# Written-out lists for the first four iterations of a fused convolution and two-layer-pair kernel, with block 2's taps summed on GpSimd

## What is computed

```python
w = softmax(weight_gen over its 7 taps)            # per token and head
x = sum over k of w[..., k] * x_pad[token - 6 + k] # causal, per head of 24 columns
h = x @ w_in                                       # 192 -> 2048
P = a0 + a1*h + a2*h**2 + a3*h**3
Q = 1 + |b0|*|h| + |b1|*h**2
x = (P / (Q + 1e-6)) @ w_out                       # 2048 -> 192
xn = x / sqrt(mean(x*x) + 1e-6) * rms_g
g, v = xn @ w_gate, xn @ w_val                     # 192 -> 1536 each
out = (silu(g) * v) @ w2_out                       # 1536 -> 192
```

## Time and profile before

| | before |
|---|---|
| median of 3 runs | 1414.27 us (1414.18 to 1414.41) |
| the profiled execution's own time | 1415.13 us |
| its span, first to last instruction | 1413.3 us |
| granted TensorE clock, mean | 0.996 |
| PE busy | 1390.0 us (98%) |
| DVE busy | 1166.2 us (83%) |
| ACT busy | 1068.9 us (76%) |
| POOL busy | 378.2 us (27%) |
| chain that ended last | PE 91%, DVE 6%, ACT 2% |

### The profile page before, as it was taken

How to read it: one execution, slowest core, us unless ns; L and a number is a source line. 1 busy time by engine, 2 the same in 40 slices (tenths; PEclk the granted TensorE clock), 3 DMA queues, 4 the chain that set the end, 5 groups by cost and what they waited for, 6 DMA issues and landing times.

```text
span 1413.3 us, 21338 instructions
## 1 busy us (share of the span) xinstructions
PE 1390.0 (98%) x7488; PEld 1247.9 (88%) x7488; DVE 1166.2 (83%) x1521; ACT 1068.9 (76%) x1388; POOL 378.2 (27%) x273
## 2 busy tenths in 40 slices
PE   7979999999999999999999999999999999999999
PEld 6858889899898998989898988989999899898988
DVE  8999988888797888888888888888879788888622
ACT  5887879878787877878787787987878787777521
POOL 3331332404233240332414133240423324000000
PEclk9999999999999999999999999999999999999999
DMA  8301000000000000000000100000000000000000
GB/s 231 90 0 32 2 32 13 32 12 0 31 11 31 11 7 35 0 31 11 31 11 0 42 0 31 11 31 11 0 31 11 31 11 1 12 1 1 12 12 12
DMA packets 12661, 32.35 MB, mean 23 GB/s; under 512 B 1620, under 2 KB 7506, under 8 KB 12624
## 3 DMA queue, kind: packets, MB, share of 16 engines
q1 hardware_dynamic: 11744, 31.42, 7.1%
q10 hardware_dynamic: 880, 0.43, 0.1%
HBM read 25.55 MB, written 6.29 MB: 23 GB/s over the span
## 4 chain that ended last, share of the span: by engine, by line
PE 91%; DVE 6%; ACT 2%; issue 0%; DMA 0%; ACTq 0%; DVEq 0%
PE dn L775 40%; PE bank L766 10%; PE bank L767 10%; PE bank L768 10%; PE bank L769 10%; PE bank L770 10%; PE bank L784 2%; DVE num L688 1%; DVE num L701 1%; DVE num L685 1%; DVE den L696 1%; DVE den L686 1%; DVE num L707 1%; ACT num L547 0%; ACT seed L558 0%
## 5 line engine op out<-in xcount | busy, mean ns | idle before, releaser
L775 PE MATMUL dn<-dn_w,num 128*128 128x192 f32 x2048 | 374.4, 327 | 5.5 <-DVE num L707 5.5
L775 PEld LDWEIGHTS dn<-dn_w,num 128*128 128x128 f32 x2048 | 340.1, 190 | 12.1 <-DVE num L707 6.7
L545 ACT ACTIVATE den<-bank,coef 128x512 f32<-128x512 f32 x256 | 175.8, 687 | 175.9 <-PE bank L770 166.9
L775 PE MATMUL dn<-dn_w,glu 128*128 128x192 f32 x1536 | 279.6, 326 | 0.0
L685 DVE TENSOR_TENSOR num<-num,bank 128x512 f32<-128x512 f32 x256 | 174.7, 682 | 106.9 <-ACT num L547 105.8
L775 PEld LDWEIGHTS dn<-dn_w,glu 128*128 128x128 f32 x1536 | 255.0, 190 | 4.0
L701 DVE SCALAR_TENSOR_TENSOR num<-num,coef,seed 128x1024 f32<-128x1024 f32 x128 | 166.9, 1305 | 56.2 <-ACT seed L568 55.7
L547 ACT ACTIVATE num<-bank,coef 128x512 f32<-128x512 f32 x256 | 200.0, 781 | 0.0
L686 DVE SCALAR_TENSOR_TENSOR den<-den,coef,bank 128x512 f32<-128x512 f32 x256 | 189.6, 741 | 0.0
L688 DVE SCALAR_TENSOR_TENSOR num<-num,coef,bank 128x512 f32<-128x512 f32 x256 | 189.6, 741 | 0.0
L732 DVE TENSOR_TENSOR glu<-glu,bank 128x512 f32<-128x512 f32 x192 | 130.8, 681 | 66.1 <-PE bank L770 64.8
(11 more groups left out here) (126 smaller groups left out, 2028.3 us busy)
## 6 DMA issues: line engine op xcount, KB each, us to landing
x_in<-in_x_dram SPq DMA_DIRECT2D x14, 960.0 KB
out_dram<-y_out SPq DMA_DIRECT2D x15, 384.0 KB, 2.3
w_blk<-in_weight_gen_dram SPq DMA_DIRECT2D x14, 112.0 KB, 2.0
dn_w<-in_moe_w_out_dram SPq DMA_DIRECT2D x1, 1536.0 KB, 10.9
dn_w<-in_moe_w_out_dram SPq DMA_DIRECT2D x1, 1152.0 KB, 18.2
num<-in_moe_w_in_dram SPq DMA_DIRECT2D x1, 768.0 KB, 7.9
num<-in_moe_w_in_dram SPq DMA_DIRECT2D x2, 384.0 KB, 9.0
x_in<-in_x_dram SPq DMA_DIRECT2D x1, 768.0 KB
```

What stands on the lines that cost most here:

```text
L545: act.activation(chunk(den, c % 8), h, ACT.Abs, scale=B_RAW[:, 1:2])
L775: done = pe.matmul(banks[:, j // 2, j % 2 * D:(j % 2 + 1) * D], acts[:, j * P:(j + 1) * P], w, start=first and j % 2 == 0, stop=last, skip ...
```

## The change

- Iterations 0 to 3 get lists of their own (`PE_OPENING` and so on). The loop's lists start at iteration 4, and lose what only the opening used. An entry `up1 4 0 < up1 0 0` is step `up1` 4 of block 0, which waits until the bank's content `up1` 0 of block 0 is read.
- Block 2's taps are no longer added by PE: POOL adds them, and two `xpose` steps follow.
- `w_first` is loaded by SP's queue ahead of x, no longer by ACT's. SP no longer waits for x or for the zeros before it issues the weights' loads. The zeros of the halo are written by DVE for block 0 and by POOL for block 1, in one partition at a time.
- ACT issues its small loads after the first exponential.
- The low part of piece 3 moves from DVE to POOL (`third_low`), with a semaphore of its own, for which `up1` 4 of block 0 waits. The first `mul` no longer waits for all low parts, but comes after `third_low` in POOL's order.
- `up1` 0 of each block starts with x's first low part and waits for the second in front of its fourth matmul.

`DVE_PROGRAM`, `UP1_BANK`, `GATE_BANK` and the loop's order of what is kept are the same.

```diff
-tap1 0 0, down1 10 2, down2 1 3, down1 11 2, down2 2 3, value 3 3, gate 5 3, up1 4 1, value 4 3, up1 5 1,
-tap1 1 0, down1 12 2, down2 3 3, down1 13 2, value 5 3, up1 6 1, tap1 2 0, tap2 0 0, gate 6 3, up1 7 1, tap1 3 0,
-tap2 1 0, down2 4 3, down1 14 2, down2 5 3, down1 15 2,
-value 6 3, gate 7 3, value 7 3, gate 8 3, up1 8 1, tap1 4 0, tap2 2 0, up1 9 1, tap1 5 0, tap1 6 0, tap2 3 0,
-gate 9 3, up1 10 1, tap2 4 0, down2 6 3, down1 0 1,
+ down1 10 2, down2 1 3, down1 11 2, down2 2 3, value 3 3, gate 5 3, up1 4 1, value 4 3, up1 5 1,
...
+PE_OPENING = opening("""
+up1 0 0, up1 1 0, up1 2 0, up1 3 0, up1 4 0 < up1 0 0, up1 5 0 < up1 1 0, tap 0 1, tap 1 1, tap 2 1,
+up1 6 0 < up1 4 0, up1 7 0 < up1 5 0, up1 8 0 < up1 2 0, up1 9 0 < up1 6 0, up1 10 0 < up1 7 0,
+up1 11 0 < up1 3 0, tap 3 1, tap 4 1, up1 12 0 < up1 9 0, up1 13 0 < up1 11 0, up1 14 0 < up1 10 0, tap 5 1,
+tap 6 1, up1 15 0 < up1 8 0, down1 0 0, down1 1 0, down1 2 0, down1 3 0, down1 4 0, down1 5 0,
+up1 0 1 < up1 12 0, down1 6 0, down1 7 0, up1 1 1 < up1 14 0, down1 8 0, up1 2 1 < up1 15 0, down1 9 0,
+down1 10 0, up1 3 1 < up1 13 0, down1 11 0, up1 4 1 < up1 0 1, up1 5 1 < up1 1 1, up1 6 1 < up1 4 1, down1 12 0,
+up1 7 1 < up1 5 1, down1 13 0, up1 8 1 < up1 2 1, down1 14 0, down1 15 0, up1 9 1 < up1 6 1, up1 10 1 < up1 7 1,
+down1 0 1, up1 11 1 < up1 3 1, down1 1 1, down1 2 1, xnx 0 0 < up1 10 1, xnx 1 0 < up1 8 1, down1 3 1,
+up1 12 1 < up1 9 1, up1 13 1 < up1 11 1, gate 0 0 < xnx 0 0, gate 1 0 < xnx 1 0, down1 4 1, up1 14 1 < gate 0 0,
+down1 5 1, up1 15 1 < gate 1 0, value 0 0 < up1 12 1, down1 6 1, gate 2 0 < up1 13 1, down1 7 1,
+gate 3 0 < up1 14 1, down2 0 0, gate 4 0 < gate 2 0, value 1 0 < up1 15 1, value 2 0 < value 0 0,
+value 3 0 < gate 3 0, down2 1 0, xpose 0 2 < value 2 0, xpose 1 2 < gate 4 0, gate 5 0 < value 1 0, down1 8 1,
+down2 2 0, up1 0 2 < xpose 0 2, up1 1 2 < value 3 0, up1 2 2 < gate 5 0, down1 9 1, up1 3 2 < xpose 1 2,
+down1 10 1, up1 4 2 < up1 0 2, up1 5 2 < up1 1 2, down1 11 1, down2 3 0, down1 12 1, value 4 0 < up1 3 2,
+down1 13 1, value 5 0 < up1 2 2, up1 6 2 < up1 4 2, up1 7 2 < up1 5 2, down2 4 0, down1 14 1,
+gate 6 0 < value 4 0, down2 5 0, down1 15 1, value 6 0 < value 5 0, gate 7 0 < up1 6 2, gate 8 0 < up1 7 2,
+value 7 0 < gate 6 0, value 8 0 < gate 7 0, up1 8 2 < value 6 0, down2 6 0, down1 0 2, down2 7 0, down1 1 2,
+up1 9 2 < value 8 0, gate 9 0 < value 7 0, gate 10 0 < up1 8 2, gate 11 0 < gate 8 0, value 9 0 < gate 9 0,
+value 10 0 < gate 10 0, up1 10 2 < gate 11 0, value 11 0 < up1 9 2, up1 11 2 < value 9 0, up1 12 2 < value 11 0,
+down2 8 0, down1 2 2, xnx 0 1 < up1 10 2, down1 3 2, xnx 1 1 < value 10 0, down2 9 0, down1 4 2,
+up1 13 2 < up1 11 2, up1 14 2 < xnx 0 1, up1 15 2 < xnx 1 1, xpose 0 3 < up1 12 2, down2 10 0, down1 5 2,
+down2 11 0, down1 6 2, xpose 1 3 < up1 13 2, down1 7 2, gate 0 1 < up1 14 2, gate 1 1 < up1 15 2,
+value 0 1 < xpose 0 3, gate 2 1 < xpose 1 3, gate 3 1 < gate 0 1,
+""")
+
+ACT_OPENING = opening("""
+linear 0 0, linear 1 0, linear 2 0, linear 3 0, table 0 0, abs 0 0, linear 4 0, linear 5 0, abs 1 0, root 0 0,
+square 0 0, square 1 0, linear 6 0, linear 7 0, piece 4 0, linear 8 0, linear 9 0, abs 2 0, abs 3 0, root 1 0,
+linear 10 0, linear 11 0, square 2 0, square 3 0, exp 0 2, abs 4 0, abs 5 0, linear 12 0, linear 13 0,
+linear 14 0, x_high 0 1, linear 15 0, root 2 0, x_high 1 1, square 4 0, square 5 0, abs 6 0, abs 7 0, root 3 0,
+square 6 0, linear 0 1, piece 5 0, linear 1 1, linear 2 1, linear 3 1, abs 0 1, linear 4 1, square 7 0,
+linear 5 1, abs 1 1, root 0 1, square 0 1, piece 6 0, square 1 1, linear 6 1, abs 2 1, ss 0 0, piece 7 0,
+linear 7 1, linear 8 1, linear 9 1, abs 3 1, root 1 1, linear 10 1, linear 11 1, square 2 1, abs 4 1,
+xn_high 0 0, xn_high 1 0, abs 5 1, square 3 1, root 2 1, silu 0 0, linear 12 1, silu 1 0, linear 13 1,
+linear 14 1, linear 15 1, square 4 1, silu 2 0, silu 3 0, square 5 1, silu 4 0, abs 6 1, abs 7 1, root 3 1,
+x_high 0 2, x_high 1 2, square 6 1, silu 5 0, linear 0 2, linear 1 2, linear 2 2, exp 0 3, square 7 1,
+linear 3 2, linear 4 2, linear 5 2, abs 0 2, abs 1 2, root 0 2, abs 2 2, linear 6 2, square 0 2, linear 7 2,
+silu 6 0, ss 0 1, abs 3 2, silu 7 0, square 1 2, root 1 2, silu 8 0, linear 8 2, square 2 2, square 3 2,
+linear 9 2, silu 9 0, silu 10 0, silu 11 0, abs 4 2, linear 10 2, linear 11 2, xn_high 0 1, xn_high 1 1,
+linear 12 2, abs 5 2, root 2 2, linear 13 2, linear 14 2, linear 15 2, x_high 0 3, y 0 0,
+""")
+
+DVE_OPENING = opening("""
+horner 0 0, horner 1 0, horner 2 0, horner 3 0, horner 4 0, horner 5 0, qy 0 0, py 0 0, py 1 0, newton 0 0,
+horner 6 0, horner 7 0, qy 1 0, horner 8 0, peak 0 2, newton 1 0, horner 9 0, horner 10 0, horner 11 0, py 2 0,
+qy 2 0, qy 3 0, newton 2 0, py 3 0, inverse 0 2, newton 3 0, horner 12 0, horner 13 0, horner 14 0, horner 15 0,
+x_low 0 1, qy 4 0, x_low 1 1, py 4 0, qy 5 0, newton 4 0, py 5 0, py 6 0, qy 6 0, newton 5 0, newton 6 0,
+horner 0 1, horner 1 1, horner 2 1, horner 3 1, horner 4 1, horner 5 1, qy 7 0, py 7 0, qy 0 1, newton 7 0,
+qy 1 1, py 0 1, py 1 1, horner 6 1, newton 0 1, newton 1 1, horner 7 1, xn 0 0, horner 8 1, horner 9 1,
+horner 10 1, horner 11 1, xn_low 0 0, xn_low 1 0, py 2 1, qy 2 1, newton 2 1, qy 3 1, py 3 1, horner 12 1,
+newton 3 1, horner 13 1, peak 0 3, horner 14 1, glu 0 0, horner 15 1, py 4 1, qy 4 1, py 5 1, glu 1 0, glu 2 0,
+newton 4 1, qy 5 1, glu 3 0, newton 5 1, x_low 0 2, x_low 1 2, py 6 1, qy 6 1, horner 0 2, newton 6 1,
+horner 1 2, horner 2 2, horner 3 2, horner 4 2, horner 5 2, py 7 1, qy 7 1, glu 4 0, newton 7 1, inverse 0 3,
+glu 5 0, horner 6 2, horner 7 2, py 0 2, glu 6 0, qy 0 2, newton 0 2, xn 0 1, glu 7 0, py 1 2, qy 1 2, glu 8 0,
+newton 1 2, horner 8 2, qy 2 2, py 2 2, horner 9 2, glu 9 0, glu 10 0, glu 11 0, horner 10 2, newton 2 2,
+qy 3 2, horner 11 2,
+""")
+
+POOL_OPENING = opening("""
+mul 0 1, mul 1 1, mul 2 1, mul 3 1, mul 4 1, mul 5 1, low 0 0 < newton 0 0, mul 6 1 < newton 0 0,
+less 0 2 < newton 1 0, low 1 0 < newton 1 0, norm 0 2 < newton 3 0, mul 0 2 < newton 3 0, mul 1 2, mul 2 2,
+add 1 2, low 2 0 < newton 6 0, mul 3 2 < newton 6 0, add 2 2, mul 4 2, add 3 2, low 3 0, low 4 0 < py 1 1,
+rms 0 0, low 5 0 < newton 1 1, low 6 0 < newton 1 1, mul 5 2, add 4 2, low 7 0, mul 6 2, add 5 2,
+less 0 3 < newton 3 1, add 6 2, norm 0 3 < newton 7 1, mul 0 3, mul 1 3, mul 2 3 < py 0 2, rms 0 1,
+add 1 3 < newton 0 2, mul 3 3 < qy 1 2, add 2 3 < newton 1 2, mul 4 3 < py 2 2, add 3 3 < py 2 2, mul 5 3,
+add 4 3, mul 6 3, add 5 3 < qy 3 2,
+""")
+
+OPENED = 4
...
-ONCE = ("piece", "low", "table")
-ALONE = {"tap1": 1, "tap2": 2}
-FLIPPED_IN_SUMS = (0, 1, 2)
-FROM_BLOCK = {"peak": 2, "less": 2, "exp": 2, "inverse": 2, "norm": 2,
-              "mul": 1, "add": 3, "xpose": 3, "x_high": 1, "x_low": 1}
 LAG = {(name, n): lag for name, n, lag in PE_PROGRAM}
-
-
-def run_iterations(eng, order, ops, last):
-
-    trail = max(3, max(lag for _, _, lag in order))
+BANK_BEFORE = {(name, n, blk): behind for name, n, blk, behind in PE_OPENING if behind}
+BANK_BEFORE.update({(name, n, OPENED - LAG[name, n]): behind for (name, n), behind in AT_FIRST.items()})
+PSUM_READ_BEHIND = {(name, n, blk): behind for name, n, blk, behind in POOL_OPENING if behind}
+
+
+def run_iterations(eng, first, order, ops, last):
+
+    trail = max(lag for _, _, lag in order)
 
     def iteration(i):
         for name, n, lag in order:
-            if name in ONCE:
-                there = isinstance(i, int) and i == lag
-            elif name in ALONE:
-                there = isinstance(i, int) and i - lag == ALONE[name]
-            elif isinstance(i, int):
-                there = FROM_BLOCK.get(name, 0) <= i - lag <= last
-            else:
-                there = True
-            if there:
+            if not isinstance(i, int) or i - lag <= last:
                 ops[name](i - lag, n)
 
-    for i in range(trail + 1):
-        iteration(i)
-    with eng.Fori(trail + 1, last) as i:
+    for name, n, blk, _ in first:
+        ops[name](blk, n)
+    iteration(OPENED)
+    with eng.Fori(OPENED + 1, last) as i:
         iteration(i)
     for i in range(last, last + trail + 1):
...
+        def zeros(eng, blk):
+
+            for n, q in enumerate(range(0, P, SEQ_P)):
+                eng.memset(x_in[q:q + 1, 0:(HALO - blk * SLOTS) * D], 0.0).then_inc(halo0, 1)
+                eng.wait_ge(halo0, blk * 2 + n + 1)
...
                 sp.dma_start(x_in[:, miss:XW], x_rows[:, 0:XW - miss]).then_inc(x_in_ready, 16)
-                sp.wait_ge(halo0, blk + 1)
                 for q in range(0, P, SEQ_P):
                     sp.dma_start(x_in[q + 1:q + SEQ_P, 0:miss],
                                  x_rows[q:q + SEQ_P - 1, PER * D - miss:PER * D]).then_inc(x_in_ready, 16)
 
+            sp.dma_start(w_first[:, :], w_rows[:, 0:2 * SLOTS * HK]).then_inc(wgen_first, 16)
             load_first(0)
-            sp.wait_ge(x_in_ready, x_count(0))
             for n in range(BY_DVE):
```

(71 more changed lines are left out.)

110 lines of the change are left out of this document (49 added, 61 removed).

## The result

The changed kernel takes 1430.03 us, the median of four runs (1429.59 to 1432.76), beside 1414.34 (1414.18 to 1414.71) for the kernel before in the same comparison: a ratio of 1.0115, 95% interval 1.0097 to 1.0132, 15.7 us slower. Predicted were 1419.0 us and a range of 1409 to 1425. The side was right and the size was not. The profiled execution took 1432.76 us, its span is 1431.0 us, 17.7 more than before. It is the longest of the four executions, 2.7 us above their median, and the profile after is of it.

A forecast was written before the change was run, and what follows sets the result against it. The prediction took DVE to bound the opening and PE the steady part. List waits of 3.3 us plus 1.5 for the clock made 4.8 on the span of 1413.3; with 1.0 from span to median, 1419.0 us, range 1409 to 1425.

The forecast's parts named there:

- M: Mark of three down groups at the head of iteration 4: at 233.24 before, foretold at 236.5, 3.3 later.
- The change part by part: Prediction's engine-by-engine account of the opening: DVE waits of 3.2 us, PE waits near 130 and 195.
- The two rivals of less time: Late stall closes: 1413.8, chance 0.27; PE's lighter load decides, DVE's waits not showing: about 1407, chance 0.17.
- the late stall: PE free at 194.6 waits for `glu` 8, behind `silu` 8 and root 1 of block 2; `up1` 9 starts at 197.0.
- less 0.7: 23.35: Start-up: first horner, possible at 24.1, comes 0.7 earlier by the loads' new order; 2.0 earlier than before.
- `xn_low` 1 ends at 125.0: Block 0 on DVE: first horner at 23.35, plus 93.9 us of work and 7.7 of waits.
- 134.9: Start of `up1` 14 of block 1, waiting for `silu` 0 behind root 2; PE idle about 5 us.
- 3.5 of small waits: DVE waits behind roots and squares, beside 52.5 us of work, from `horner` 12 of block 1 at 136.
- 2.04 + 1.29 + 0.6 + 0.7 = 4.6: From DVE reaching `qy` 1 of block 2 at 192 to PE's `up1` 9 of block 2: 4.6 us.
- my 0.8 for short waits: PE's short waits, 0.8 us, with the nine groups (10.3 us) from `up1` 9 of block 2.
- The clock term: Half clock on PE behind its waits in the opening: 1.5 us added, bounds 0 and 5.
- The rival that the clock stays low: PE at 1.2 GHz from 105 to 140, each wait drawing the next: 5 to 8 us more, 1425, chance 0.15.

The follow-up runs named there:

- the sums on POOL alone: The kernel before, with old lists and old start-up, but POOL adding block 2's taps, with two transposes: 1415.35 us in ten runs, ratio 1.0008.
- the repairs: Changed kernel with weights after x, newtons moved, silus ahead of roots, root's waits swapped, dummy roots, linear 6, linear 8 and rms moved ahead: 1415.0 us.
- the run with the loads alone: The kernel before with w_first first on SP's queue and the weights issued without waiting for x: 1417.02 us, ratio 1.002.
- The run with the table loaded in the wait: Changed kernel with weights after x, newtons moved, silus first, root's waits swapped, plus one-column dummy roots ahead of four roots: 1417.18 us.
- the execution with the dummies: Profiled execution of the changed kernel with 7 to 12 dummy matmuls at each of four PE waits; median 1429.71 us, ratio 1.0111.

## Why the prediction was wrong

**The place and the mechanism held.** M moved, nothing behind M did (1180.1 foretold, 1180.0 measured), and each wait named in "The change part by part" is in the trace: 3.25 and 3.24 for 3.2, 4.79 for about 5 in front of `up1` 14, one in front of `up1` 9 of block 2. That PE's relief alone is worth nothing is shown by the sums on POOL alone (+1.1, which can't be told from no change), and that the new order's waits cost the rest by the repairs, nearly all of them to the lists, which brought the time from 1430.0 to 1415.0 with PE's work unchanged. The two rivals of less time fell: DVE's waits don't hide, and the late stall grew instead of closing.

**The late stall was mis-sized.** The term "`up1` 9 of block 2 starts at 197.0" is the step that failed; it starts at 209.21. The terms that make it up were too small: the small waits on DVE, the table loads in front of the roots, and the start-up. M came 14.5 later than foretold, to which the sum had added 1.5 for the clock; in the median, below the profiled execution by 2.7, the forecast was missed by 11.0. This is how the 14.5 add up:

- Start-up, "less 0.7: 23.35". The first horner came at 25.27, 1.9 later. In this execution x landed late beside the weights. I had put the gain at 0.7 with 0 as a bound; the run with the loads alone shows a loss, 2.2 us at the first product. That case, x later than before, lay outside my bounds.
- "`xn_low` 1 ends at 125.0" was 130.3, 3.4 more than the start explains. On DVE's timeline waits of 0.85, 0.91, 0.31 and 0.47 us that I had not listed are 2.5 of it, 0.23 ahead of `qy` 4 are another part. The rest is spread over many steps.
- `up1` 14 of block 1, "134.9", came at 140.39: 5.5 late, of which nothing is new.
- "3.5 of small waits" between `horner` 12 of block 1 and `qy` 1 of block 2. DVE's timeline has 2.15 (x_low behind root 3), 2.41 and 0.19 (horner behind root 0), 0.92 (`xn` behind POOL's `rms`), 0.73, 0.56 and 0.44: 7.4. That is 3.9 more, and `qy` 1 of block 2 ended at 203.1, 11 behind my 192. The 0.92 is of the kind of the stalls: POOL's `rms` stood behind `mul` 2 of block 3, which waits for `py` 0 of block 2.
- "2.04 + 1.29 + 0.6 + 0.7 = 4.6" from there to `up1` 9 (192 and 4.6 give 196.6, not the 197.0 that I wrote) lacks a table load: I took the load in front of a root as done while ACT waits. The chain shows it as 1.10 us of issue ahead of the root at 204.53; the load itself took 1.28. The same load stood in front of the roots at 160.93 and 184.45, and so is part of the 2.15 and the 2.41 above. Root 2 of block 1 had none. The run with the table loaded in the wait gave back 4.2 us.
- Behind `up1` 9, 39.5 us to M were foretold and 41.8 measured. In the stall the clock fell: from 209.21 to 215.31 PE started fourteen matmuls, most of them 0.43 us apart, where later ones are 0.23 apart: 6.1 us for 3.2. Of these 2.9 us my 0.8 for short waits covered a part.

1.9, 3.4, 0.2, 3.9, 1.3 and 2.3 come to 13.0. The other 1.5 lie between `horner` 12 and `qy` 1. About 1.0 of them is `qy` 0 of block 2 at 194.58: it took 2.19 us where others take 1.22, beside a multiply of POOL that ran from 194.14 for 1.54. I had priced all steps undisturbed, since the new order was to keep POOL beside horners. The last 0.5 I can't place.

**The clock term is only partly settled.** 1.5 us were foretold for the whole opening. Between 84 and 140 the clock was 0.85, and up to `xn_low` 1 that was nearly free: the execution with the dummies gained 0.5 to 1.0 us there, because DVE set the pace. Where PE set it, behind 209, the half clock cost 2.9, about twice the term by itself; between 137 and 160 it cost 1.2 to 2.5 more by the one profiled execution with the dummies, and nothing by the median. The rival that the clock stays low came nearest of all with its 1425, but the repairs show that most of the loss had another cause: 15.0 us went by order, four dummy roots and the start-up, and with them the clock was still 0.68 in 84 to 100 and 0.80 in 100 to 125.

**Table loads** were weighed for the silus. In the changed kernel the load in front of `silu` 0 started 0.02 us behind the root, took 1.28, and the silu started 0.01 behind it. So the Trainium skill, "ScalarE: Activation LUTs", What ACT_TABLE_LOAD costs, with its 2.66 us for a switch is not borne out here, as I had said (and two times 1.4 on 1419 make 1421.8, not 1421.5). The weighing had me look at the length of a load and not at where it stands, and there the cost was.
